# The last 64 tokens of a v projection: high and low part side by side in TensorE's array, and the work around it reordered

## What is computed

```python
h = x @ w_in                       # x: 4 x 576 x 512, w_in: 512 x 1024
h = 0.5 * h * (1.0 + np.tanh(c * (h + 0.044715 * h ** 3)))
u, v = (h[..., :512], h[..., 512:])
v_n = (v - mu) / np.sqrt(var + 1e-06) * g_ln        # mean and variance over the 512 columns
v_s = np.einsum('ts,bsd->btd', w_sg, v_n) + b_sg[None, :, None]
x = x + (u * v_s) @ w_out
...
xn = (x - mu) / np.sqrt(var + 1e-06) * g_ln2        # next block
x = x + np.maximum(xn @ w_ch1, 0.0) @ w_ch2
```

## Time and profile before

| | before |
|---|---|
| median of 3 runs | 666.21 us (666.0 to 667.43) |
| the profiled execution | 666.58 us |
| its span, first to last instruction | 664.8 us |
| granted TensorE clock, mean | 1.000 |
| PE busy | 655.3 us, 99% |
| DVE / ACT / POOL busy | 529.1 / 356.8 / 245.9 us |

### The profile page before, as it was taken

How to read it: one execution, slowest core, us unless ns; L and a number is a source line. 1 busy time by engine, 2 the same in 40 slices (tenths; PEclk the granted TensorE clock), 3 DMA queues, 4 the chain that set the end, 5 groups by cost and what they waited for, 6 DMA issues and landing times.

```text
span 664.8 us, 14064 instructions
## 1 busy us (share of the span) xinstructions
PE 655.3 (99%) x5160; PEld 622.8 (94%) x5160; DVE 529.1 (80%) x1162; ACT 356.8 (54%) x897; POOL 245.9 (37%) x258
## 2 busy tenths in 40 slices
PE   8999999999999999999999999999999999999997
PEld 4679998999899998999999999999999999999997
DVE  5967866887679868998876885786999898898883
ACT  6866864488347844434563462345684344444440
POOL 0477240635152438468436447223001412113011
PEclk9999999999999999999999999999999999999999
DMA  8660007000530051128353667869952726517301
GB/s 296 258 241 4 1 3 278 36 1 2 186 146 2 1 176 59 56 69 291 119 171 121 199 241 251 306 216 348 303 171 84 290 72 246 165 58 282 90 19 53
DMA packets 49924, 98.25 MB, mean 148 GB/s; under 512 B 4673, under 2 KB 33217, under 8 KB 47297
## 3 DMA queue, kind: packets, MB, share of 16 engines
q1 hardware_dynamic: 49152, 96.16, 42.2%
q0 software_dynamic: 704, 1.21, 0.8%
HBM read 64.83 MB, written 32.52 MB: 146 GB/s over the span
## 4 chain that ended last, share of the span: by engine, by line
PE 89%; DVE 4%; issue 2%; ACT 2%; POOL 2%; DVEq 0%; POOLq 0%; ACTq 0%
PE pair L1886 17%; PE pair L1888 17%; PE pair L1887 17%; PE pair L1677 9%; PE pair L1679 9%; PE pair L1678 9%; PE pair L1701 3%; PE pair L1734 3%; PE pair L1716 3%; ACT probs L1026 1%; DVE stage L1546 1%; PE pair L1685 1%; DVE res L1406 1%; DVE acc_a L489 1%; PE pair L1797 1%
## 5 line engine op out<-in xcount | busy, mean ns | idle before, releaser
L1886 PE MATMUL pair<-xf_hi,w_hi 128*128 128x288 f32 x896 | 265.6, 296 | 0.2
L1887 PE MATMUL pair<-xf_lo,w_hi 128*128 128x288 f32 x896 | 264.5, 295 | 0.0
L1888 PE MATMUL pair<-xf_hi,w_lo 128*128 128x288 f32 x896 | 263.6, 294 | 0.0
L1888 PEld LDWEIGHTS pair<-xf_hi,w_lo 128*128 128x128 f32 x896 | 168.8, 188 | 0.0
L1886 PEld LDWEIGHTS pair<-xf_hi,w_hi 128*128 128x128 f32 x896 | 167.9, 187 | 0.8 <-ACT rstd L1103 0.7
L1887 PEld LDWEIGHTS pair<-xf_lo,w_hi 128*128 128x128 f32 x896 | 168.2, 188 | 0.0
L1131 ACT ACTIVATE xf_hi<-res 128x576 fp32r<-128x576 f32 x140 | 94.3, 683 | 89.1 <-PE pair L1888 71.9
L1546 DVE TENSOR_TENSOR stage<-pair,stage 128x576 f32<-128x576 f32 x136 | 100.7, 752 | 39.5 <-PE pair L1888 33.3
L567 DVE TENSOR_TENSOR xf_lo<-res,xf_hi 128x576 fp32r<-128x576 f32 x140 | 109.8, 793 | 14.7 <-ACT xf_hi L1131 14.2
L1012 POOL TENSOR_TENSOR xr<-xr,stage 128x576 f32<-128x576 f32 x16 | 32.9, 2058 | 165.7 <-DVE stage L1546 165.6
L1223 ACT ACTIVATE stage<-stage 128x576 f32<-128x576 f32 x64 | 43.6, 683 | 79.8 <-DVE stage L1546 79.7
(11 more groups left out here) (134 smaller groups left out, 1285.0 us busy)
## 6 DMA issues: line engine op xcount, KB each, us to landing
hid_scratch<-stage SPq DMA_DIRECT2D x64, 288.0 KB, 3.5
res<-hid_scratch SPq DMA_DIRECT2D x16, 1152.0 KB, 6.8
w_raw<-w_ff_dram SPq DMA_DIRECT2D x16, 512.0 KB, 4.2
v_sb<-vW_dram SPq DMA_DIRECT2D x16, 384.0 KB, 6.7
xr<-x_scratch SPq DMA_DIRECT2D x16, 288.0 KB, 3.0
out_dram<-xr SPq DMA_DIRECT2D x16, 288.0 KB, 3.3
k_sb<-kT_dram SPq DMA_DIRECT2D x15, 304.0 KB, 6.3
q_sb<-qT_dram SPq DMA_DIRECT2D x15, 288.0 KB, 6.2
```

What stands on the lines that cost most here:

```text
L1886: pe.matmul(dst, wh, xh, start=(start and x == 0), stop=False)
L1887: pe.matmul(dst, wh, xl, start=False, stop=False)
L1888: last = pe.matmul(dst, wl, xh, start=False, stop=(stop and x == n - 1))
```

## The change

- `xop_hi` and `xop_lo` become the two halves of one tensor `xop`. POOL copies the last 64 tokens of both, chunk by chunk, side by side into the memory of `vn_hi` of the last group, which is free then (`place_short`, 4 copies of 128x128 elements a batch).
- The last v group is two passes a chunk: the 128 stationary columns are 64 high and 64 low ones, by `win_hi` and by `win_lo`. That is 8 matmuls in place of 12. The result lies in two halves of bank 0: rows 0 to 63 from the high parts and rows 64 to 127 from the low ones.
- ACT copies the low half out, DVE adds the high half (`add_short`), and ACT applies the gelu twice, once to the upper and once to the lower rows of the tile (`gelu_short`), one behind the other.
- The remainder of the last normalised group goes from POOL to DVE (`split_last_v`).
- ACT applies the gelus of v before the squares, which follow the fourth and the fifth group. The last sum of squares goes from DVE to POOL, behind `split_all_v`. The first copy of the variance goes ahead of the last `sum_hi`.
- In the last period both `split_first` go behind `norm_all_v`. On SP one store of a hidden tile goes ahead of the loads of the eighth unit of weights.

```diff
+            def place_short(b, pair):
+                pool.wait_ge(x_lo, b * PAIRS + (pair + 1))
+                if b >= 1:
+                    pool.wait_ge(group_ready, (b - 1) * len(GROUPS) + NGELU + NMIX)
+                pool.tensor_copy(xshort[:, pair, :, :],
+                                 xop[:, :, pair, S - LAST:S]).then_inc(x_short, 1)
...
             def split_all_v(b):
                 root_v(b, 0)
-                for s in range(NS):
-                    if s + 1 < NS:
-                        root_v(b, s + 1)
+                for s in range(NS - 1):
+                    root_v(b, s + 1)
                     split_v(b, s)
...
                 split_all_v(b)
+                if b >= 1:
+                    sum_chunks(pool, 4 * (b - 1) + 3)
...
+                act.activation(gv[0:LAST, s, :], bank[GROUP_BANK[s]][LAST:P, :], ACT.Copy).then_inc(short_copied, 1)
+
+            def gelu_short(b):
+                s = NS - 1
+                act.wait_ge(short_added, b + 1)
+                act.activation(gv[LAST:P, s, :], gv[0:LAST, s, :], ACT.Gelu_apprx_tanh).then_inc(short_doubled, 1)
+                act.wait_ge(short_doubled, b + 1)
+                act.activation(gv[0:LAST, s, :], gv[0:LAST, s, :], ACT.Gelu_apprx_tanh).then_inc(gelu_done, 1)
...
-                if norm and not last:
-                    for h in range(2):
-                        squares(n, h)
                 for s in range(NS):
                     gelu_v(b, s)
+                    if norm and not last and s >= NS - 2:
+                        squares(n, s - NS + 2)
                     if first and s >= NS - 2:
                         split_wsg(2 * s - 2 * NS + 4)
                         split_wsg(2 * s - 2 * NS + 5)
+                gelu_short(b)
...
                     if b >= 1 and t == 0:
+                        copy_variance(b - 1, 0)
                         sum_hi(4 * b - 1)
...
-                    if b >= 1 and t == 0:
-                        copy_variance(b - 1, 0)
...
+            def add_short(b):
+                x = gv[0:LAST, NS - 1, :]
+                dve.wait_ge(short_copied, b + 1)
+                dve.tensor_tensor(x, bank[GROUP_BANK[NS - 1]][0:LAST, :], x, ALU.add).then_inc(short_added, 1)
+
+            def split_last_v(b):
+                dve.wait_ge(vnh_ready, (b + 1) * NS)
+                dve.tensor_tensor(vn_lo[:, NS - 1, :], gv[:, NS - 1, :], vn_hi[:, NS - 1, :].bitcast(F32),
+                                  ALU.subtract).then_inc(vnl_ready, 1)
...
                     if s >= 1:
                         v_norm(b, s - 1)
+                    if s == 1:
+                        add_short(b)
...
                         sum_chunk(dve, 4 * (b - 1) + 2, s)
+                split_last_v(b)
...
                     split_sum(dve, 4 * n + 2)
-                    sum_chunks(dve, 4 * n + 3)
...
+                norm_all_v(b)
                 for g in range(2):
                     split_first(dve, g)
-                norm_all_v(b)
-                for g in range(2):
                     split_rest(dve, g)
...
-                    pe.wait_ge(x_lo, b * PAIRS + (k + 1))
+                    pe.wait_ge(x_short if s == NS - 1 else x_lo, b * PAIRS + (k + 1))
+                    if s == NS - 1:
+                        for w in (win_hi, win_lo):
+                            last = pe.matmul(bank[GROUP_BANK[s]], vn_hi[:, NS - 1, k * P:(k + 1) * P], w[:, k, GATE:],
+                                             start=(k == 0 and w is win_hi), stop=(k == KC - 1 and w is win_lo))
+                        continue
```

More of the change, by code:

```diff
@@ L206, in sequence_block_kernel @@
         win_lo = sb("win_lo", [P, KC, 2 * GATE], F32R, phase_a)
-        xop_hi = sb("xop_hi", [P, KC, S], F32R, phase_a)
-        xop_lo = sb("xop_lo", [P, KC, S], F32R, phase_a)
+        xop = sb("xop", [P, 2, KC, S], F32R, phase_a)
+        xop_hi, xop_lo = xop[:, 0, :, :], xop[:, 1, :, :]
         wsg_hi = sb("wsg_hi", [P, NS, S], F32R, phase_a)
@@ L218, in sequence_block_kernel @@
         vn_hi = sb("vn_hi", [P, NS, GATE], F32R, phase_a)
+        xshort = vn_hi[:, NS - 1, :].rearrange("p (k i t) -> p k i t", k=KC, i=2)
         mask_b = sb("mask_b", [P, 3, P], BF16, phase_a)
@@ L312, in sequence_block_kernel @@
         x_act, x_dve = sem("x_act"), sem("x_dve")
-        x_hi, x_lo = sem("x_hi"), sem("x_lo")
+        x_hi, x_lo, x_short = sem("x_hi"), sem("x_lo"), sem("x_short")
         group_ready = sem("group_ready")
         gelu_done = sem("gelu_done")
+        short_copied, short_added, short_doubled = sem("short_copied"), sem("short_added"), sem("short_doubled")
         bn_done, aggr_done = sem("bn_done"), sem("aggr_done")
@@ L761, in _ @@
             save_x(B - 1)
[L762 to L765, removed]
+            load_raw(UNITS - 2)
+            load_first(UNITS - 2)
+            load_rest(UNITS - 2)
+            store_hidden(0, 1, 0)
+            load_raw(UNITS - 1)
+            load_first(UNITS - 1)
+            load_rest(UNITS - 1)
             for n in range(B):
@@ L784, in _ @@
                         load_rest(UNITS + 2 * q - 1)
-                    store_hidden(m, 1, 0)
+                    if m > 0:
+                        store_hidden(m, 1, 0)
                     if m == 12:
@@ L847, in split_x @@
                                    ALU.subtract).then_inc(x_lo, 1)
+                if b == 0:
+                    place_short(b, pair)
+            def place_short(b, pair):
[4 more added lines that the diff above has]
+                                 xop[:, :, pair, S - LAST:S]).then_inc(x_short, 1)
             def root_v(b, s):
@@ L938, in period @@
                         split_x(b + 1, QUAD_X[t])
+                    for pair in {4: (0, 1), 6: (2,), 7: (3,)}.get(t, ()):
+                        place_short(b + 1, pair)
                     if b >= 1 and t == 2:
@@ L968, in _ @@
             split_x(0, 2)
-            pool.wait_ge(x_lo, PAIRS)
+            place_short(0, PAIRS - 1)
             for c in range(1, KC):
@@ L1062, in gelu_v @@
             def gelu_v(b, s):
+                if s < NS - 1:
+                    act.wait_ge(group_ready, b * len(GROUPS) + (s + 1))
+                    act.activation(gv[:, s, :], bank[GROUP_BANK[s]], ACT.Gelu_apprx_tanh).then_inc(gelu_done, 1)
+                    return
                 act.wait_ge(group_ready, b * len(GROUPS) + (s + 1))
[L1065 to L1068, removed]
+                act.activation(gv[0:LAST, s, :], bank[GROUP_BANK[s]][LAST:P, :], ACT.Copy).then_inc(short_copied, 1)
[5 more added lines that the diff above has]
+                act.activation(gv[0:LAST, s, :], gv[0:LAST, s, :], ACT.Gelu_apprx_tanh).then_inc(gelu_done, 1)
             def gelu_u(b, g):
```

## The result

The changed kernel takes 668.84 us (median of 22 runs, 666.77 to 670.78); the kernel before, measured beside it, takes 667.47 us (median of 22 runs, 666.0 to 669.49; of the three runs shown ahead of the prediction, which are among them, two lie at the lower end). The ratio is 1.0019, 95% interval 1.0011 to 1.0027: **1.3 us slower**, between 0.7 and 1.8. The profiled run took 670.78 us, the longest of the 22, with a span of 669.0 (before: 664.8) and a mean granted clock of 0.997 (before: 1.000).

The account below looks back on a forecast made before the run. PE, busy 99% of the span, was taken as the bound. Period 0 +2.6, periods 1 and 2 -2.2 and period 3 -0.2 gave +0.2 us on 666.2, written as 666.3; own range 665.0 to 667.5, 80% range 662.4 to 668.3.

Parts of the forecast that it names:

- Removed from PE: Last v group: four matmuls fewer a period save PE 0.91 us each period, 3.65 us over four.
- Periods 1 and 2: No collision there as in period 0; each wins 0.91 us, with the transpose wait of period 2 together -2.2 us.
- the 0.43 of the transpose: Period 2: PE's 0.4 us wait at a transpose goes, as the copy of the variance now stands ahead of sum_hi.
- Period 0, the ring gets later: Chain from gelu to vn_lo: add_short blocks DVE's queue, shifting it some 1.2 us; fourth vn_lo ends at 55.5.
- Period 0, strict turns, and the cast takes one: DVE and POOL alternate through four wout_lo, cast included, until 62.5; mix group 0 waits 3.5 us, period 0 2.6 longer.
- Rivals 1 and 2: Period 0: wait about 2 us or less, 664.9 us, chance 0.17; no new wait, 662.1 or 663.0 us, chance 0.17.
- Period 3: Mix 0 1.1 us sooner; out group 4 loses 0.1, out group 6 0.8; 0.2 is left, bounds 0 and 1.1.
- The sum: Whole kernel: +2.6 for period 0, -2.2 for periods 1 and 2, -0.2 for period 3, together +0.2 us.
- the new wait: PE at mix group 0 of period 0: arrives at 58.99, waits 3.5 us for DVE's last remainder, ending near 62.5.
- rival 3: Clock falls to 1.2 GHz in period 0's pause: +1.9 to +3.7 us for mix groups, 668.2 to 670.0, chance 0.12.
- The level: Starting time of the kernel before: 666.2 us by the median, its profiled execution of 666.58 being 0.4 above.

Follow-up runs that it names:

- e3: Changed kernel with the add of the two short parts behind the second v_norm, not the first, in period 0: 668.30 us, ratio 1.0019 to the kernel before.
- e1: Changed kernel with GpSimd's four w_out remainders in period 0 waiting until VectorE's last w_sg remainder is done: 664.65 us, ratio 0.9956 to the kernel before.
- e10: e1 with ACT's first copy of the variance in periods 1 and 2 behind the second rounding again: 664.91 us, ratio 0.9956.
- e13: e1 with the second sums of periods 1 and 2 on VectorE again: one run of 663.99 us.
- e14: e1 with both the sums on VectorE and ACT's copy of the variance behind the rounding again: one run of 664.22 us.
- e2: Changed kernel with 24 idle matmuls on TensorE ahead of mix group 0's wait in period 0: 667.26 us, ratio 0.9993 to the kernel before.
- e9: e1 with period 3's two 128x512 weight remainders in VectorE's idle places ahead of the v statistics: 664.38 us, ratio 0.9946 to the kernel before.
- e8: e1 with GpSimd's weight sums for blocks 2 and up in period 3 waiting for VectorE's second normalisation: 665.37 us, ratio 0.9973.
- e4: Changed kernel with the fifth v remainder on GpSimd again in all periods, ahead of the w_out remainders: 665.16 us, ratio 0.9970.
- e15: The kernel of e9 unchanged, measured a second time: 662.75 us, ratio 0.9949 to the kernel before.

## Why the prediction was wrong

- **Removed from PE**: right. Periods 1 and 2, where nothing else interferes, are shorter by 0.95 and 1.42 us, against 0.91 and, with the 0.43 of the transpose, 1.34 forecast.
- **Period 0, the ring gets later**: right in size (fourth `vn_lo` ends at 55.42, forecast 55.5), half right in reason, as e3 shows: 0.6 of it is the add's own work.
- **Period 0, strict turns, and the cast takes one**: right. Every end is within 0.2 us of the forecast (55.7, 57.2, 58.9, 60.6 and 62.4 for 55.8, 57.3, 59.1, 60.8 and 62.5), and e1 shows the whole of it as the neighbour's doing. Mix 0 came at 62.48 for 62.5, a wait of 3.43 us for 3.5. Rivals 1 and 2 are out. The Trainium skill, "SBUF — State Buffer", section "Who interferes with whom", counts a cast among the instructions that can hold the port pair that VectorE shares with GpSimd. This trace agrees: 1.42 us beside `wout_lo`, where e1, with GpSimd idle, has 0.43.
- **Periods 1 and 2**: right, except for whose merit the 0.4 us is: not the copy's new place alone, either of two moves (e10, e13, e14).
- **Period 3**: mix 0 came 1.05 us sooner (forecast 1.1). The loss at out group 6 is 0.78 (forecast 0.8), that at out group 4 is 0.26 (forecast 0.1); the three cancel, and with 0.1 us spread over the rest the period ends at +0.1 instead of -0.2, just outside the bounds given. That the losses came out near the forecast is partly luck: the sum took for granted that VectorE meets GpSimd on the way as in the kernel before. With the other outcome of the tie (e2, e3) group 4 loses nothing and group 6 0.53, and the period is 0.5 us shorter than before.
- **The sum: the step that failed is the price of the new wait.** It went in at its own length, with nothing for TensorE's clock behind it; that was left to rival 3, to which I gave 0.12. "Nothing shows a fall either, and scores run until shortly before" was no reason against it: a trace whose longest wait behind the first 38 us is 0.4 us says nothing of one eight times as long. The runs show the clock at half speed behind the wait, for 14 steps of 0.24 us in the profiled one, at a cost of 1.5 us, and a mean clock below 0.999 in 20 of 22. e2 takes the pause away, leaves VectorE's chain as late, and gets the 1.5 us back. With that term my sum is +1.7, against 1.8 in the profile and 1.3 (0.7 to 1.8) measured. 1.5 is less than the 1.9 to 3.7 of rival 3, but that is one execution: the runs with a mean of 0.997 and of 0.995 lie 1.9 and 3.1 us above the two with 1.000. The Trainium skill, "TensorE: Matmul & The Clock Gate", section "What's actually happening", says that idling puts the array back to its slow state. This trace agrees: 0.50 behind the wait of 3.43 us, 1.00 in its place with 24 fillers.
- **The level**: three runs put the kernel before at 666.21 us, 22 runs at 667.47. Half of the distance from 666.3 to 668.84 is this, half the change.

## What to carry to other kernels

Price a new wait on TensorE as the wait plus what the clock does behind it: here 3.4 us of waiting cost 4.9 in all, and the second part shows only in the matmuls' spacing and in the granted clock of short stretches. When a step leaves GpSimd's queue, look at what moves up into the gap and whom it meets on VectorE; here one constant wait on GpSimd turned a 1.3 us loss into a gain of 3. Where an engine has many short idle places ahead of a critical chain, small independent work is better placed there than behind the chain (0.89 us in e9). And before an edit is credited with half a microsecond of one profiled execution, look whether two engines met in another order far from the edit (e8).

## What the runs showed of the hardware

- TensorE's clock fell after it stood still for 3.43 us (mean clock 0.997 or less in 20 of 22 runs) and 2.9 us (10 of 12), and not after 1.6 us (11 of 12). A single mean of 0.996 or 0.997 also turned up among 29 runs of the kernel before, 6 of e1, 12 of e4 and 12 of e8, which have no such pause; those runs have no trace. A mean of 0.999 need not be a fall in the work: in the profiled e1 the clock falls only behind the last matmul (granted clock 1.00 until 659 us, 0.75 from there to the end at 661.7). In the changed kernel it fell behind the pause, while TensorE was busy again: at 64.0 us, 1.5 us after mix 0 began.
- A cast of 128x512 to fp32r takes 0.43 us with GpSimd idle (e1) and 1.42 beside a GpSimd tensor_tensor of 128x512; the difference is the wait for GpSimd's turn.
- Of two remainders that VectorE and GpSimd start 0.03 us apart, GpSimd's went first in 11 of 14 profiled executions and VectorE's in three (e2, e3, e8), with the same code at that place. Going second cost VectorE 0.64 us (1.39 for 0.75).
- The same kernel's feed-forward part took 363.18 us in one execution and 360.95 in another (e9, e15), with waits of VectorE for a `stage` buffer's DMA of 7.1 and 4.5 us in all; single profiled spans differ by this much without any cause in the edit.
